# Placing every wide SBUF tensor of a fused attention and two-layer FFN kernel on a multiple of 64 bytes

## The reference

```python
scores = scale * np.matmul(q, k.transpose(0, 1, 3, 2)) + bias     # masked to 8 + 96 keys
a = softmax(scores);  x = np.matmul(a, v)                         # as (1536, 512)
h = x @ w_in;         solu = h * softmax(h)
y = layer_norm(solu) * g_ln @ w_out
yn = y / sqrt(mean(y * y) + 1e-6) * rms_g
out = (silu(yn @ w_gate) * (yn @ w_val)) @ w_down
```

## Time and profile before

| | us |
|---|---|
| median of 3 executions | 598.04 (596.92 to 598.3) |
| span of the profiled execution | 596.7 |
| TensorE matmul busy in it | 566.4 (95%) |
| VectorE, ScalarE, GpSimd busy | 305.0, 258.1, 74.6 |

### The profile page before, as it was taken

How to read it: one execution, slowest core, us unless ns; L and a number is a source line. 1 busy time by engine, 2 the same in 40 slices (tenths; PEclk the granted TensorE clock), 3 DMA queues, 4 the chain that set the end, 5 groups by cost and what they waited for, 6 DMA issues and landing times.

```text
span 596.7 us, 10660 instructions
## 1 busy us (share of the span) xinstructions
PE 566.4 (95%) x3696; PEld 511.4 (86%) x3696; DVE 305.0 (51%) x786; ACT 258.1 (43%) x597; POOL 74.6 (13%) x215
## 2 busy tenths in 40 slices
PE   2488999999999999999999999999999999999997
PEld 1477888888888888878899999999999999999996
DVE  5478788777877898868455223222222222231211
ACT  2566756655665677646454212221222222222112
POOL 1240220222112205213010010001001000100000
PEclk9998799999999999999999999999999999999999
DMA  7676464433443343232532100010020000000000
GB/s 171 185 192 163 132 182 125 121 101 101 124 113 103 105 126 96 83 135 82 176 109 93 49 23 2 1 70 1 1 70 0 0 0 35 0 0 36 2 1 36
DMA packets 22965, 46.95 MB, mean 79 GB/s; under 512 B 4128, under 2 KB 4128, under 8 KB 22928
## 3 DMA queue, kind: packets, MB, share of 16 engines
q1 hardware_dynamic: 22928, 46.48, 26.8%
HBM read 40.18 MB, written 6.29 MB: 78 GB/s over the span
## 4 chain that ended last, share of the span: by engine, by line
PE 78%; DVE 9%; DMA 3%; issue 3%; POOL 3%; ACT 2%; SPq 1%; ACTq 0%; DVEq 0%
PE hidden L396 9%; PE hidden L397 8%; PE hidden L398 8%; PE mixed L1211 5%; PE mixed L396 3%; PE mixed L397 3%; PE scores_b L396 3%; PE scores_b L397 3%; PE scores_b L398 3%; PE mixed L398 3%; PE turned L396 3%; PE turned L397 3%; PE scores_a L397 3%; PE turned L398 3%; PE scores_a L396 3%
## 5 line engine op out<-in xcount | busy, mean ns | idle before, releaser
L708 ACT ACTIVATE act_hi<-act_sb 128x256 fp32r<-128x256 f32 x72 | 30.1, 418 | 108.7 <-DVE act_sb L1070 108.7
L1211 PEld LDWEIGHTS mixed<-v_in,probs_t 116*128 116x128 f32 x384 | 55.3, 210 | 14.5 <-ACT probs_t L659 10.8
L1211 PE MATMUL mixed<-v_in,probs_t 116*128 116x64 f32 x384 | 54.2, 289 | 9.8 <-ACT probs_t L659 9.8
L1070 DVE TENSOR_TENSOR act_sb<-mixed,silu 128x256 f32<-128x256 f32 x36 | 15.3, 425 | 93.7 <-PE mixed L398 93.1
L1070 DVE TENSOR_TENSOR act_sb<-turned,silu 128x256 f32<-128x256 f32 x36 | 15.3, 424 | 89.0 <-PE turned L398 86.5
L396 PE MATMUL hidden<-down_hi,act_hi 128*128 128x512 f32 x144 | 57.0, 396 | 0.1
L397 PE MATMUL hidden<-down_lo,act_hi 128*128 128x512 f32 x144 | 56.9, 395 | 0.0
L398 PE MATMUL hidden<-down_hi,act_lo 128*128 128x512 f32 x144 | 56.7, 394 | 0.0
L659 ACT ACTIVATE probs_t<-turned 116x512 f32<-116x512 f32 x48 | 28.7, 597 | 60.7 <-PE turned L1196 60.7
L1075 DVE TENSOR_TENSOR act_lo<-act_sb,act_hi 128x256 fp32r<-128x256 f32 x72 | 30.6, 425 | 34.9 <-ACT act_hi L708 34.9
L649 ACT ACTIVATE probs<-logits,neg_max 128x232 f32<-128x232 f32 x96 | 45.7, 482 | 5.8 <-DVE neg_max L961 5.8
(11 more groups left out here) (140 smaller groups left out, 1537.2 us busy)
## 6 DMA issues: line engine op xcount, KB each, us to landing
qk_raw<-qk_pairs SPq DMA_DIRECT2D x96, 180.0 KB, 3.5
v_in<-v_windows SPq DMA_DIRECT2D x12, 464.0 KB
staging<-w_gate SPq DMA_DIRECT2D x3, 1024.0 KB, 6.5
staging<-w_val SPq DMA_DIRECT2D x3, 1024.0 KB, 5.5
y_spill<-y_out SPq DMA_DIRECT2D x12, 256.0 KB, 8.4
staging<-w_down SPq DMA_DIRECT2D x3, 1024.0 KB, 5.5
y_in<-y_spill SPq DMA_DIRECT2D x6, 512.0 KB, 3.7
out<-o_sb SPq DMA_DIRECT2D x12, 256.0 KB, 2.1
```

The costliest lines, as they stand in the source:

```text
L708: nc.scalar.activation(act_hi[:, slot], act_sb[:, slot], ACT.Copy).then_inc(act_rounded, 1)
L1070: nc.vector.tensor_tensor(act_sb[:, slot], val_ps[slot][:, 0:WIDE], silu[:, slot], ALU.mult).then_inc(act_ready, 1)
L1211: ins = pe.matmul(mixed[:, head * d:(head + 1) * d], probs_t[:, p % 2, h, half], v_in[:, even, half, head * d:(head + 1) * d], start=(half ...
```

## The change

The helper that places an SBUF tensor looks at where the tensor would start. If its last dimension is 128 or more and the start is an odd multiple of 32 bytes, it places an unused tensor of 32 bytes ahead of it. No instruction, wait, transfer or loop differs.

```diff
+SBUF_BYTES = 224 * 1024 - 32
+HALF_LINE = 32
...
         def sbuf(ctx, name, shape, dt=F32):
+            if shape[-1] >= P and (SBUF_BYTES - nc.sbuf_bytes_remaining + HALF_LINE - 1) // HALF_LINE % 2:
+                ctx.enter_context(nc.sbuf_tensor(f"before_{name}", [P, HALF_LINE // 4], F32))
             return ctx.enter_context(nc.sbuf_tensor(name, shape, dt))
```

## The result

The changed kernel takes 600.91 us in the median of 6 executions (600.54 to 602.07), the kernel before 598.6 (596.92 to 599.75, 6 runs that include the three shown above). The ratio is 1.0043, with a 95% interval of 1.0028 to 1.0059: 1.7 to 3.5 us slower. The forecast was 596.0, the range 593.0 to 598.8.

The account below looks back on a forecast made before the run. TensorE was taken to bound the kernel, with VectorE's chain in part of stage one. Savings of 1.6 (block 1 weights) and 0.4 (scores) made 2.0 us, taking the median 598.04 to 596.0, range 593.0 to 598.8.

Parts of the forecast that it names:

- odd to even: Tensor starts moving from odd multiples of 32 bytes to multiples of 64 shorten matmul distances; chance 0.60.
- Block 1 of gate and value: Stage two, steps 4 to 7: its weights moving to multiples of 64 save 1.6 us over 6 blocks of tokens.
- third rival: Loaded and streamed starts equal within 512 bytes lengthen distances; steps 0-3 and 8-11 lose 3.3 us, time 601.4; chance 0.09.
- The scores: Stage one: loaded `qk_hi` moving to a multiple of 64 speeds 192 matmuls, 0.4 us saved, bounds 0 and 0.6.
- 512 columns: Matmuls of this width, as in `narrow`: no effect of starts, bounds plus and minus 1 ns by 432, 0.4 us.
- Streamed `yt`: Stage two, 1,728 matmuls of 256 columns: moving the streamed start taken to save 0; other bound 5.0 us.
- second rival: The streamed side pays for odd starts as the loaded one does: 5.0 us more comes off, 591.0; chance 0.10.
- `probs_t`, `v_in`, the transfers: 384 float32 matmuls, taken at 0, other bound 1.1 us; transfers, mainly the first wait, 0, bounds 0 and 0.5.
- first rival: Place low or high in memory, not the start within 64 bytes, sets distances: no gain, 598.0; chance 0.21.

Follow-up runs that it names:

- e3: Changed kernel with `yt_hi` and `yt_lo` alone moved 32 bytes further up, back on an odd multiple of 32: 597.13 us, 0.9973 of the kernel before.
- m1: TensorE alone repeats a 256-column matmul, loaded start swept in 32-byte steps, streamed start fixed: 117.1 to 119.4 ns by loaded start less streamed start, within 256 bytes.
- m4: TensorE alone, 8 loaded by 8 streamed starts within 256 bytes crossed, at 256 and 512 columns; 512 columns with equal starts took 226.7 to 229.2 ns.
- e1: Kernel before with `yt_hi` and `yt_lo` alone moved by 32 bytes to a multiple of 64: 598.61 us, ratio 0.9993.
- e2: Kernel before with `gate1` and `val1` alone moved by 32 bytes to a multiple of 64: 598.85 us, ratio 0.9998.
- e4: Kernel before with gate and value blocks 0, 1, 2 padded to odd multiples of 32, at differences +64, +128, 0 from `yt`: 600.75 us, ratio 1.0031.
- e5: Kernel before with 32-byte pads ahead of hi and lo parts of gate and value, blocks 0 and 1: 599.07 us beside 598.08, one execution each.
- e6: Changed kernel with `yt` alone moved, so gate and value weights stand 64 bytes above it within 256: 596.3 us, 0.9963 of the kernel before.
- e7: As e6, with 160 bytes placed ahead of `staging` so all from there on stand 128 bytes further up: 595.76 us, 0.9955 of the kernel before.
- m3: TensorE alone, loaded start swept over 2,048 bytes: 512 columns took 227.3 to 233.7 ns a matmul, 232 columns 111.5 to 112.1.

## Why the prediction was wrong

**The step that failed** is the reading of the earlier trace rows: "odd to even" was taken as the cause of the longer distance in steps 4 to 7, with a chance of 0.60. The rows showed two things that differed at once between block 0 and block 1, the loaded start by itself and its difference to `yt`, and `yt` was odd throughout. The cause is the difference: e3 changes it and leaves the weights' starts and places alone, and in m1 to m4 the pace follows it. With the curve of m1 the gate and value matmuls of a block can be worked out for each kernel, as 24 a step by the distance. Changes against the kernel before, in us a block (second to fifth):

| kernel | gate and value by the curve | gate and value measured | `narrow` measured | whole block |
|---|---|---|---|---|
| after | 8 steps from 117.1 to 119.2: +0.40 | +0.59 | -0.07 | +0.52 |
| e1 | 8 steps to 117.6, 4 from 119.2 to 117.1: -0.11 | -0.19 | 0.00 | -0.19 |
| e2 | 4 steps to 118.1: -0.11 | -0.13 | +0.03 | -0.11 |
| e3 | 4 steps to 117.1: -0.20 | -0.22 | -0.11 | -0.33 |
| e4 | 4 steps to 117.9, 4 to 118.8, 4 to 119.2: +0.24 | +0.20 | +0.02 | +0.22 |
| e5 | by each matmul's own pair: -0.01 | +0.09 | -0.07 | +0.03 |
| e6, e7 | 8 steps from 117.1 to 117.9, 4 from 119.2 to 117.9: +0.03 | -0.01 | -0.37 | -0.38 |

For gate and value the sign is right wherever the curve gives more than 0.03, and the size to within 0.10 but in the changed kernel, whose runs stand at 120.0 ns where the sweep has 119.2. For `narrow` the sweep of 512 columns gives no such account: by it the changed kernel, e3, e6 and e7 should all gain the same 0.17 (32 of a block's 72 matmuls, those that stream `down1` or `down2_lo`, go from difference +32 to 0, 5.3 ns each), and they gained 0.07, 0.11, 0.37 and 0.37. Stage two as a whole grew by 2.98 us, and less the 0.48 us ahead of it that is the growth of the span.

**Block 1 of gate and value, 1.6 us gained:** nothing was. Weights and `yt` both moved by 32, so the difference stayed 0. What was not in the sum at all are the other 8 steps: 6 blocks by 8 steps by 24 is 1,152 matmuls, whose weights moved by 64 and whose stream by 32. The third rival had that term at 3.3 us; gate and value together grew by 0.59 us a block, 3.5 for six. It gave 601.4 for the 600.91 measured.

**Why the rival got 0.09.** It was put off with the scores, whose starts leave unlike rests and which had the larger surplus over their columns. m3 shows that 232 columns take 111.5 to 112.1 ns wherever the loaded operand stands, so the scores could say nothing on 256. The surplus of one width was carried over to another. The rival's own period of 512 bytes was wrong as well: it is 256. For the changed kernel both give difference 0 everywhere, so its time came out right all the same.

**The scores, 0.4 us gained:** no. The three distances of the earlier trace rows, 340 ns there, take 336 ns before and 337 after in the median of the 48 pairs, not the 321 of "107 apart". By m3 at most 0.6 ns by 192 is to be had, 0.1 us.

**512 columns, 0 with bounds of 1 ns:** too tight. The earlier trace rows compare differences of -32 and 0 through single stretches of five distances, and the runs of the kernel before and after mix these with other work. In `narrow` the change made all differences 0, and a run went from 1.38-1.40 to 1.39 us, 1.393 to 1.388 in the mean; in e6 and e7, at the same differences, it takes 1.36, which over six blocks is 2.2 us, far beyond the bound of 0.4. The runs of `ffn_in` fell from 1.482 to 1.473 us (middle three quarters of 46 runs in each trace), the direction that m3 gives. In e7, with the same differences, they took 1.478, so this one is not settled.

**Streamed `yt`, 0, and the second rival:** the streamed start by itself gave no 5 us. That the streamed tensor's start matters is true, but by the sweeps in relation to the loaded one.

**`probs_t`, `v_in`, the transfers:** taken at 0. The seven distances within eight matmuls of `mix_pair` took 0.727 us before and after (medians of 48), the transfers kept their times to landing to 0.1 us but for `w_val` (5.5 to 6.4 us; 5.4 to 6.9 in the other runs of the kernel), and the first row of stage two moved by less than the spread between executions. No loss or gain is shown there, nor tested by itself.

**The first rival, "not the start within 64 bytes":** rightly seen that the kernel before could not tell start from place; e3 rules place out. The rule of the Trainium skill that stood beside it ("SBUF — State Buffer", "Specifications (TRN2)", lines of 16 bytes) would have given no change; the runs differ by up to 6 ns in 233 between starts that are all on lines of 16 bytes.

**The bounds.** The upper ends of the list that the range rests on add up to 5.7 us, not 5, so by its own terms the range would have begun near 592.3. The measured time lies beyond the other end.

## What to carry to other kernels

An aligned start isn't good in itself: what TensorE's pace depends on here is where the loaded operand starts relative to the streamed one within 256 bytes, and the good difference depends on the width (0 for 512 columns repeated alone, not 0 for 256). It is not the whole rule: inside the kernel 512 columns at difference 0 took 231.3, 230.7 and 227.1 ns in the mean with `yt` at three starts, so a placement has to be tried in the kernel itself and read group by group. Where a trace offers two groups that differ in two properties at once, move one tensor alone before believing either; in e3 `yt` moved by 32 bytes, and 0.43% slower became 0.27% faster. And a rival should be dismissed only by rows of the same shape: 232 columns proved nothing about 256.

## What the runs showed that was not expected

- The distance of float32r matmuls of 256 columns runs from 117.1 to 119.4 ns with the difference of the starts, period 256 bytes, and down to 113.6 in a few places; 512 columns take 227.3 ns at difference 0 and 230.1 to 233.7 elsewhere.
- 232 columns are flat (111.5 to 112.1 ns), 24 columns short of a width that is not.
- The same difference can run at two paces in steady repetition (1.37 and 1.41 us for 12 in e4, 1.36 and 1.41 in e1), and two alternating pairs of starts run at 116.9 to 117.2 ns where each held constant gives 118.7 to 119.4. What in the chip meets, and when, no run here shows.
- Moving `yt` changed the pace of matmuls that do not read it: `narrow` went from 16.61 us a block in e3 to 16.35 in e6.
- Padding alone, with no instruction changed, moves this kernel between 595.76 and 600.91 us, 0.9%.
